# Moving VectorE's preparation steps and one value tile in a fused attention, token/channel mixer and gated feed-forward kernel

## What is computed

```python
a = softmax([local scores in a window of 16 | scores on 24 block maxima of k]) @ [v | block means of v]
h = relu(xt @ w_tok1) @ w_tok2;  u = x + h.T          # mixer over tokens
x = u + relu(u @ w_ch1) @ w_ch2                       # mixer over channels, 1536 hidden
xk = mu_k * x + (1 - mu_k) * x_prev
xr = mu_r * x + (1 - mu_r) * x_prev
out = sigmoid(xr @ w_r) * (relu(xk @ w_k) ** 2 @ w_v) # 1024 hidden
```

## Time and profile before

| | us |
|---|---|
| runs: median (lowest to highest) | 488.78 (487.01 to 489.02) |
| profiled execution, its own time | 486.57 |
| its span | 484.8 |
| PE busy | 459.0 (95% of the span) |
| DVE busy | 331.2 (68%) |
| ACT busy | 258.2 (53%) |
| POOL busy | 217.3 (45%) |

### The profile page before, as it was taken

How to read it: one execution, slowest core, us unless ns; L and a number is a source line. 1 busy time by engine, 2 the same in 40 slices (tenths; PEclk the granted TensorE clock), 3 DMA queues, 4 the chain that set the end, 5 groups by cost and what they waited for, 6 DMA issues and landing times.

```text
span 484.8 us, 7812 instructions
## 1 busy us (share of the span) xinstructions
PE 459.0 (95%) x2848; PEld 410.3 (85%) x2848; DVE 331.2 (68%) x700; ACT 258.2 (53%) x529; POOL 217.3 (45%) x213
## 2 busy tenths in 40 slices
PE   5889899999999999999999899889999989999997
PEld 4777777788999999999999799878888868988885
DVE  6799998487766666448767786658889762586403
ACT  5799997455433233422453246157677862676510
POOL 6656774342236633654247525624644364063000
PEclk9999999999999999999999999999999999999999
DMA  6999944310212121212121212112121214310003
GB/s 169 269 241 231 210 104 71 131 43 1 87 45 85 46 87 45 88 56 75 51 82 52 79 43 88 44 44 87 45 87 45 87 43 154 108 45 1 1 0 130
DMA packets 45441, 41.20 MB, mean 85 GB/s; under 512 B 20832, under 2 KB 36704, under 8 KB 45408
## 3 DMA queue, kind: packets, MB, share of 16 engines
q1 hardware_dynamic: 45408, 40.78, 30.3%
HBM read 37.62 MB, written 3.15 MB: 84 GB/s over the span
## 4 chain that ended last, share of the span: by engine, by line
PE 74%; ACT 9%; DVE 6%; issue 5%; DMA 2%; POOL 2%; SPq 0%; ACTq 0%; DVEq 0%; POOLq 0%
PE bank L1327 18%; PE bank L1329 18%; PE bank L1328 18%; PE bank L1464 12%; PE bank L1465 6%; ACT e_sb L642 4%; DMA v<-in_v_dram 2%; ACT qbd L622 2%; DVE ucF L1056 1%; ACT kt L630 1%; DVE w1L L1025 1%; POOL xL L546 1%; DVE rL L1148 1%; DVE c L1143 1%; PE bank L1397 1%
## 5 line engine op out<-in xcount | busy, mean ns | idle before, releaser
L1327 PE MATMUL bank<-ucH,w1H 128*128 128x384 f32 x280 | 94.7, 338 | 6.0 <-DVE c L1143 1.7
L1329 PE MATMUL bank<-ucH,w1L 128*128 128x384 f32 x280 | 94.0, 336 | 0.0
L1328 PE MATMUL bank<-ucL,w1H 128*128 128x384 f32 x280 | 94.0, 336 | 0.0
L572 POOL TENSOR_TENSOR w1S<-stg 128x256 f32<-128x256 f32 x20 | 17.9, 894 | 148.7 <-PE bank L1329 148.7
L1327 PEld LDWEIGHTS bank<-ucH,w1H 128*128 128x128 f32 x280 | 52.6, 188 | 13.4 <-issue 7.4
L586 POOL TENSOR_TENSOR w2L<-stg,w2H 128x512 fp32r<-128x512 f32 x40 | 58.9, 1494 | 1.6
L786 ACT ACTIVATE rH<-c 128x384 fp32r<-128x384 f32 x36 | 18.9, 526 | 69.4 <-DVE c L1143 69.4
L1328 PEld LDWEIGHTS bank<-ucL,w1H 128*128 128x128 f32 x280 | 52.9, 189 | 2.3
L1329 PEld LDWEIGHTS bank<-ucH,w1L 128*128 128x128 f32 x280 | 52.6, 188 | 0.0
L1329 PE MATMUL bank<-w2H,rL 128*128 128x512 f32 x96 | 37.9, 395 | 0.0
L1328 PE MATMUL bank<-w2L,rH 128*128 128x512 f32 x96 | 37.9, 395 | 0.0
(11 more groups left out here) (147 smaller groups left out, 1169.5 us busy)
## 6 DMA issues: line engine op xcount, KB each, us to landing
stg<-in_moe_w_ch_dram SPq DMA_DIRECT2D x24, 512.0 KB, 3.4
stg<-in_moe_w_k_dram SPq DMA_DIRECT2D x8, 512.0 KB, 3.5
stg<-in_moe_w_v_dram SPq DMA_DIRECT2D x8, 512.0 KB, 3.5
vw<-in_v_dram SPq DMA_DIRECT2D x16, 240.0 KB, 4.8
kn<-in_k_dram SPq DMA_DIRECT2D x8, 384.0 KB, 5.6
qn<-in_q_dram SPq DMA_DIRECT2D x8, 384.0 KB, 6.8
v<-in_v_dram SPq DMA_DIRECT2D x8, 384.0 KB, 5.2
stg<-in_moe_w_tok_dram SPq DMA_DIRECT2D x6, 256.0 KB, 4.3
```

What stands on the lines that cost most here:

```text
L1327: pe.matmul(dst, wH, mH, start=start, stop=False, **more)
L1328: pe.matmul(dst, wH, mL, start=False, stop=False, **more)
L1329: return pe.matmul(dst, wL, mH, start=False, stop=stop, **more)
```

## The change

Three things are moved; nothing is added or removed.

1. The tables of `ahead` are rewritten from quad 7 on: in quads 7 to 12 nothing is left at place 2. In quads 13 to 16 place 2 keeps one step each, in 17 to 19 none. Place 3 is used from quad 7 on.
2. In quad 12 the additions `wide(1, 0)`, `wide(1, 1)` and `side(1, 1)` come later in DVE's order.
3. One value tile moves from the gap after P1 to the gap after P3, and each gap after the first takes its tiles one earlier in the list. `gate` waits for the low half of xr by one block before each block, in place of four blocks before the first.

```diff
         T_AT = {(1, 0): (3,), (2, 0): (4,), (3, 0): (5,), (4, 0): (6,),
-                (9, 1): (3, 4), (9, 2): (5, 6), (14, 1): (3, 4), (14, 2): (5, 6)}
+                (8, 3): (3, 4), (9, 1): (5, 6), (14, 1): (3, 4), (14, 2): (5,), (14, 3): (6,)}
...
-                (10, 1): (0, 1), (10, 2): (3,), (11, 1): (4, 5), (11, 2): (6, 2),
-                (14, 3): (0,), (15, 1): (1, 3), (15, 2): (4, 5), (15, 3): (6, 2)}
+                (9, 3): (0, 1), (10, 1): (3,), (10, 3): (4, 5), (11, 1): (6,), (11, 3): (2,),
+                (14, 3): (0,), (15, 1): (1, 3), (15, 2): (4,), (15, 3): (5, 6, 2)}
...
-        MIX_AT = {(7, 1): ((0, 0), (1, 0)), (7, 2): ((2, 0), (3, 0)), (8, 1): ((0, 1), (1, 1)), (8, 2): ((2, 1), (3, 1)),
-                  (13, 1): ((0, 0), (1, 0), (2, 0)), (13, 2): ((3, 0), (0, 1), (1, 1)), (13, 3): ((2, 1), (3, 1))}
+        MIX_AT = {(7, 1): ((0, 0), (1, 0), (2, 0)), (7, 3): ((3, 0), (0, 1), (1, 1)), (8, 1): ((2, 1), (3, 1)),
+                  (13, 1): ((0, 0), (1, 0), (2, 0)), (13, 2): ((3, 0),),
+                  (13, 3): ((0, 1), (1, 1), (2, 1), (3, 1))}
...
+        XR_AT = {(8, 3): (4,), (9, 1): (5,), (10, 1): (6, 7), (10, 3): (0,), (11, 1): (1, 2), (11, 3): (3,),
+                 (17, 1): (0, 1), (17, 3): (2, 3), (18, 1): (4, 5), (18, 3): (6, 7)}
+        XR_SPLIT_AT = {(16, 1): (0, 1), (16, 2): (2,), (16, 3): (3,), (17, 3): (0, 1), (18, 1): (2, 3),
+                       (18, 3): (4, 5), (19, 1): (6, 7)}
...
                 ahead(q, 1)
-                if q == NQ:
-                    wide(1, 0)
                 plus(P7, u3, Bk, p1)
...
                 if q == NQ:
-                    wide(1, 1)
+                    wide(1, 0)
                 plus(P4, c21, Bk, p1)
...
-                if q == NQ:
-                    side(1, 1)
                 plus(P3, c12, A, u2)
                 low_k(R21, 1, 0, c21)
                 if q == NQ:
+                    wide(1, 1)
+                    side(1, 1)
                     wide(1, 2)
...
-                    if st % RT == 0:
-                        pe.wait_ge(xrl_done, 8 * b + KT * (st // RT + 1))
...
+                        if st % RT == 0:
+                            pe.wait_ge(xrl_done, 8 * b + KT * (st // RT) + kk + 1)
...
-            TILE_GAPS = (range(0, 2), range(2, 3), range(3, 5), range(5, 6), range(6, 8), range(8, 10), range(10, 12))
+            TILE_GAPS = (range(0, 1), range(1, 2), range(2, 4), range(4, 5), range(5, 7), range(7, 9), range(9, 12))
```

More of the change, by code:

```diff
@@ L311, in build_program @@
         T_AT = {(1, 0): (3,), (2, 0): (4,), (3, 0): (5,), (4, 0): (6,),
-                (9, 1): (3, 4), (9, 2): (5, 6), (14, 1): (3, 4), (14, 2): (5, 6)}
+                (8, 3): (3, 4), (9, 1): (5, 6), (14, 1): (3, 4), (14, 2): (5,), (14, 3): (6,)}
         U_AT = {(1, 1): (0,), (2, 1): (1,), (3, 1): (3,), (4, 1): (4,), (4, 2): (5,), (5, 1): (6,), (5, 2): (2,),
-                (10, 1): (0, 1), (10, 2): (3,), (11, 1): (4, 5), (11, 2): (6, 2),
-                (14, 3): (0,), (15, 1): (1, 3), (15, 2): (4, 5), (15, 3): (6, 2)}
-        MIX_AT = {(7, 1): ((0, 0), (1, 0)), (7, 2): ((2, 0), (3, 0)), (8, 1): ((0, 1), (1, 1)), (8, 2): ((2, 1), (3, 1)),
-                  (13, 1): ((0, 0), (1, 0), (2, 0)), (13, 2): ((3, 0), (0, 1), (1, 1)), (13, 3): ((2, 1), (3, 1))}
-        XR_ORDER = (4, 5, 6, 7, 0, 1, 2, 3)
[L321 to L325, removed]
+                (9, 3): (0, 1), (10, 1): (3,), (10, 3): (4, 5), (11, 1): (6,), (11, 3): (2,),
[3 more added lines that the diff above has]
+                  (13, 3): ((0, 1), (1, 1), (2, 1), (3, 1))}
+        XR_ORDER = (4, 5, 6, 7, 0, 1, 2, 3)
+        XR_AT = {(8, 3): (4,), (9, 1): (5,), (10, 1): (6, 7), (10, 3): (0,), (11, 1): (1, 2), (11, 3): (3,),
+                 (17, 1): (0, 1), (17, 3): (2, 3), (18, 1): (4, 5), (18, 3): (6, 7)}
+        XR_SPLIT_AT = {(16, 1): (0, 1), (16, 2): (2,), (16, 3): (3,), (17, 3): (0, 1), (18, 1): (2, 3),
+                       (18, 3): (4, 5), (19, 1): (6, 7)}
         def set_ahead(q):
```

## The result

The changed kernel takes **482.82 us** (median of 6 runs, 482.56 to 483.07) against 487.81, the median of six runs of the kernel before, the prediction's three among them: ratio 0.9896, 95% interval 0.9878 to 0.9914. That is 5.0 us, where 3.1 were forecast. The sign was right and the size was not. The forecast of 485.7 started from 488.78; of the 2.9 between it and 482.82, 1.0 is this other base. The profiled execution took 482.56, its span is 480.8.

The account below looks back on a forecast made before the run. PE was taken as the bound, with DVE and POOL waiting for each other second. 9.80 us of pauses go and 6.73 come, net -3.1 from 488.78: 485.7 us, forecast's own range 484.1 to 487.3, stated range 482.5 to 489.4.

Parts of the forecast that it names:

- What bounds, and what goes: PE bounds; its pauses from quad 7 to the wait before the gate sum to 9.80 us, and all go.
- The line of DVE and POOL: DVE instructions with both inputs in SBUF and POOL's take turns: P5 of quads 9-11 1.7 late together, P7 of 14, 18 1.44 each.
- rival 1: Instructions in line cost what they do alone, so P5 and P7 are later: no net change, 489.2 us; chance 0.22.
- rival 2: DVE slips between POOL's instructions, P5 and P7 on time: 481.1 us; chance 0.16 with all between it and the forecast.
- Quad 19: Like quads 15 and 16: u2 begins by 4.9 after P1's start (T) at the latest, 0.3 early, so no loss.
- rival 3: u2 bounds every quad with tiles, P7 late in quads 15, 16 and 19 too: +4.8, 493.5 us; chance 0.12.
- Quad 16 and the gate: The gate's wait for xrL (2.15) goes but is given back; quad 16 to 17 stays 34.36.
- the middle between a won and a lost race: Quad 16: R12's low half or POOL's first low half of w_r goes first; 0.70 gained or lost, middle taken.
- the store: Later steps, stores included, hang on POOL's second low half of w_r up to the fourth sigmoid and quad 17; gives back 2.15.
- -9.80 + 6.73: Whole sum: 9.80 us of pauses go, 1.7 + 1.44 + 1.44 + 2.15 come; net -3.1.
- The forecast's lower bound: Net -4.7 us: the race at quad 16 won, and quads 10 and 11 without a loss.
- The 115 ns: Skill page's delay before the blocked side goes on; at some 50 handovers, 5.9 us on top of the sum, 491.6.

Follow-up runs that it names:

- lost on purpose: Changed kernel with ACT's first high half of w_r in quad 16 put ahead of p1, so POOL's low half is ready before R12's: 484.08 us, ratio 0.992.
- the wait alone: Kernel before with only the gate's wait for xrL made block by block: ratio 0.9962 of the kernel before, -1.4 us.
- experiment 1: Parts alone on the kernel before: tables with quad 12's additions 0.9946, moved tiles 0.9969, gate's wait for xrL 0.9962, quad 12's additions 0.9937.

## Why the prediction was right or wrong

- **What bounds, and what goes**: right. All pauses before P1 are gone, P4 of quad 12 is on time, and the wait for xrL before the gate is gone.
- **The line of DVE and POOL**: right, and so were its prices. P5 of quads 9 to 11 costs 0.92, 0.32 and 0.52, 1.76 together, where 1.7 were forecast (the single ones were 1.0, 0.1 and 0.6, so their sum is closer than they are); P7 of quads 14 and 18 costs 1.50 and 1.46, where 1.44 were. With the prices of instructions alone (rival 1) quad 14 would have lost 2.2. DVE was let through nowhere (rival 2).
- **Quad 19**: wrong by 0.47. The prediction said that in quads 15, 16 and 19 u2 begins by T + 4.9. The trace before already spoke against it, since there u2 of quad 19 began 5.01 after P1, with one mixing and one low half ahead, where the change puts two of each (P1, then u2):

```profile
441.01 0.34 PE L1327 MATMUL bank<-ucH,w1H 128*128 128x384 f32 x1
...
446.02 0.55 DVE L1205 TENSOR_TENSOR u<-bank,p 128x384 f32<-128x384 f32 x1
```

  In quads 15 and 16 it held (T + 3.1 and T + 4.4). In quad 19 POOL has no sums left and waits for the last value tile of quad 17, which comes just before P1. DVE's steps up to u2 (two low halves of xr, between, left out), then POOL's cast:

```profile
437.42 2.38 DVE L1103 SCALAR_TENSOR_TENSOR xrF<-u,mu,xrF 128x384 f32<-128x384 f32 x2 [1.75 <-ACT xrF L762]
...
441.75 0.55 DVE L1210 TENSOR_TENSOR rL<-c,rH 128x384 fp32r<-128x384 f32 x1
442.22 0.55 DVE L1205 TENSOR_TENSOR u<-bank,p 128x384 f32<-128x384 f32 x1
...
436.78 1.04 POOL L582 CAST w2H<-stg 128x1024 fp32r<-128x1024 f32 x1 [11.51 <-PE bank L1327]
```

  P1 is at 436.54, the cast 0.24 behind it, u2 at P1 + 5.68, beyond the 5.23 from which the prediction had P7 late. It is rival 3's mechanism, at one of its three places.
- **Quad 16 and the gate**: this is the step that failed; by itself it is more than the whole miss, of which quad 19 takes some back. The prediction took "from quad 16 to quad 17 the same 34.36 as before, so the 2.15 is given back by the store". Measured is 32.29. Two things were put together there. One was the middle between a won and a lost race, 0.70 each way: the race was won, and lost on purpose it costs 1.41, so its size was right and 0.70 of the miss comes from taking the middle where one side came true. The other 1.4 is the store: the prediction held that all steps from POOL's second low half of w_r to the fourth sigmoid come in the same distances as before, and that this sigmoid sets quad 17. These are the sixth gate tile on PE and the stores on SyncE's queue, before and then after:

```profile
406.83 0.41 PE L1327 MATMUL bank<-WrH,xrH 128*128 128x512 f32 x1
...
399.58 12.00 SPq L434 DMA_DIRECT2D out_dram<-sg  x6
...
400.98 0.39 PE L1325 MATMUL bank<-WrH,xrH 128*128 128x512 f32 x1
...
394.75 10.90 SPq L434 DMA_DIRECT2D out_dram<-sg  x6
```

  Before, the fourth sigmoid ended at 406.68 and the sixth tile, the one that needs it, began 0.15 behind it without being held up; I took the sigmoid's long wait for the tile's. From the end of POOL's low half to the start of the sigmoid it was 14.35 then and is 11.96 now (387.19 to 399.15): the first store was issued 0.3 sooner in this count and landed 4.4 after its issue instead of 6.5. So nothing waited, neither with the gate 1.3 earlier (the wait alone, 11.75) nor with the change. An estimate from these rows: any landing up to some 5.6 would have left the sixth tile on time, and with the 6.5 of before it would have been 0.9 late. That the store landed sooner was not foreseen, and its cause is open. The term measured -2.07: the gate begins behind POOL's second low half of w_r, 15.83 after quad 16's P1.
- **The sum**: -9.80 + 6.73 became -9.80 + 5.2, that is -4.6 from quad 7 on. Of the miss of 1.5, the gate is 2.07 and quad 19 is 0.47 the other way. The medians, 5.0 apart here and 6.0 when the changed kernel was run again, hold more than that; the profiles can't say where it lies, but the first stretch varies by more. The forecast's lower bound comes out as -4.5 by its own two terms, not -4.7. By its size the result fell into what was given to rival 2 and the times up to the forecast (0.16), though rival 2's mechanism is nowhere to be seen.
- **The page of the Trainium skill**: the exclusive lock (SBUF — State Buffer, "SBUF: two separate sides") is borne out (5.42 against 2.55 for the same four mixings, 2.75 against 0.55 for the same low half). The 115 ns (SBUF — State Buffer, "A bandwidth-pool intuition that's wrong") are stated there for a DMA whose descriptors GpSimd writes; that they follow each handover was the prediction's reading. Between these instructions they are not seen: seven of them behind one another take 4.9, while alone they take 4 x 0.53 + 1.04 + 2.54 = 5.7.

## What to carry to other kernels

Where two engines can't run together, a step costs by what it meets: count, for every instruction that the bounding engine waits for, all instructions of both engines between the line's start and it, at the price they have in line. Then spread the movable steps so that no such line reaches its due time; emptying one place altogether only moves the queue. And a long wait that ends just as the bounding engine needs the result is not yet a bound, nor is its length fixed: a DMA in its chain can take 2 us less in the next kernel. Move the start of the stage alone, as experiment 1 does, and see whether the end moves with it.

## What the runs showed of the hardware

An instruction that was held up by the other engine takes a smaller share of such a line than its length alone: 0.92 for POOL's cast against 1.04, 1.15 for w2L against 1.27, 0.44 for a mixing against 0.53. The smaller figures are worked out from lines of several instructions, not read off a single one. The turn goes to the one that waits. At quad 16 DVE's low half of R12 began 0.04 us before POOL's low half in both profiles of the changed kernel, and went through in 0.55; begun 0.33 after it, it took 2.75.

The first store landed 4.0 to 4.9 us after its issue in the eight profiles whose gate waits block by block and whose store has the load of 512 KB ahead of it, and 5.2 to 6.5 in the four whose gate waits for four blocks first. Behind the store instead of ahead of it, the same load took the store off ACT's path. Why the landing differs was not tried.
